# Score products of a windowed attention on quarters of the array, with queries stored plainly instead of as block-diagonal head pairs

## The chip, the cores and the metric

The kernel runs on one core of one Trainium2 chip. Times are device microseconds of one execution; the figure that counts is the median over several runs. A profiled execution gives the trace; its times count from the span's start.

## The reference, cut to what matters

Three layers follow one another: windowed attention, a layer of 8 experts of which each token uses 2, and a dense layer with 2048 hidden columns. The change touches the attention alone.

```python
# q, k, v: batch 4, 8 heads, 576 positions, 64 values a head
scores = scale * np.matmul(q, k.transpose(0, 1, 3, 2))
rel = pos[:, None] - pos[None, :]
mask = (rel >= 0) & (rel < 64)
scores = np.where(mask, scores, -1000000000.0)
scores = scores - np.max(scores, axis=-1, keepdims=True)
attn = np.exp(scores)
attn = attn / (np.sum(attn, axis=-1, keepdims=True) + 1e-09)
return np.matmul(attn, v)
```

## The kernel before

The 576 positions are 9 blocks of 64. A query of block i sees only keys of blocks i-1 and i, so a step s works on one block i = s // 4 of one batch b = s % 4 with all 8 heads: 36 steps. The 8 heads are 4 pairs (J = 4). Heads of a pair lie one above the other: the 64 values of the one on partitions 0 to 63, those of the other on 64 to 127. Queries and keys come transposed, so partitions are what a score product sums over.

A step's scores are one PSUM bank of 128 x 512: for pair j columns 128j to 128j+127 hold the 128 keys (two blocks of 64), and partitions hold 64 queries of the one head and 64 of the other. `scores(s)` (L917) first writes the mask there by a bf16 product with an identity (L932), then adds 4 fp32 products of full size (L936). For these to keep the heads apart, the stationary operand `q_bd` is block-diagonal: queries of the first head on partitions 0 to 63 and columns 0 to 63, of the second on partitions 64 to 127 and columns 64 to 127, and zeros elsewhere. VectorE writes the zeros once (L684, L685, four fills; the semaphore `zeroed`), and the loads fill in only the two diagonal parts.

TensorE's queue is written out by hand and works in order. In step s it does the scores of step s (L932, L936), transposes the probabilities of step s-2 (`transposed_probs`, L947), multiplies those of s-3 with the values (`values`, L959: 8 products of 64 stationary columns, going to output partitions 0 to 63 and 64 to 127 by turns), transposes the result of s-4 (`transposed_x`, L969), and in every second step forms the routing logits (`logits`, L978). VectorE takes the row maxima (L699), copies the transposed probabilities (L710) and scales the result (L723); ScalarE takes the exponentials (L552). Both also prepare the first expert's weights. Three banks hold scores, so the scores of step s wait for the exponentials of step s-3.

Queries come over SyncE's queue: block 0 in three parts by batch (0, 1, and 2 with 3), each as one transfer for either head (L289), then block 1 (`load_q`, L255, again two transfers a block), then keys. `q_bd` holds two blocks. ScalarE's queue loads the keys of blocks 0 and 1 in the same three parts (L569), and first values between them (L573). A part is complete when `row0_loaded` has counted its transfers. Before its first scores TensorE runs 12 filling products (L909).

Behind attention come routing on VectorE, gathers by GpSimd, then the expert and dense layers, whose products fill TensorE to the end.

Of the kernel before, what the change touches and what calls it, by code (L numbers as in the profile page):

```python
# [27 lines left out]
P = 128  # L28
# [17 lines left out]
def build(nc, qT, kT, vW, noise, w_gate, w_noise, w1, w2, w_in, w_out, out):  # L46
    BLOCKS, _, B, JQ = qT.shape
    Q = 64
    J = JQ // Q
# [6 lines left out]
    CH = 3  # L56
# [24 lines left out]
    with ExitStack() as ctx:  # L81
# [35 lines left out]

        with ExitStack() as s1:
            sb = sb_in(s1)
            q_bd = sb("q_bd", [P, 2, B, J, 2, Q])  # L120
            k_ring = sb("k_ring", [P, 4, B, JQ])
            v_ring = sb("v_ring", [P, B, D])
            probs = sb("probs", [P, CH, JQ * 2])
            probsT = sb("probsT", [P, J * P])
            xT_blk = sb("xT_blk", [P, 2, 2, 2, Q])
            negmax = sb("negmax", [P, 4, J])
            bias = sb("bias", [P, 4, J])
            rowsum = sb("rowsum", [P, 8, J])
            rowsum_g = sb("rowsum_g", [P, 2, J])
            rowinv = sb("rowinv", [P, 2, J])  # L130
            mask_first = sb("mask_first", [P, P], BF16)
            mask_odd = sb("mask_odd", [P, P], BF16)
            mask_even = sb("mask_even", [P, P], BF16)
            ident_b = sb("ident_b", [P, P], BF16)
            w_gn = sb("w_gn", [P, KD, 2 * E])
            x_blk = sb("x_blk", [P, CH, 2, JQ])
# [113 lines left out]
        @block.sync  # L250
        def _(sp):
            def load_q(r):
                for hi in range(2):
                    rows = slice(64 * hi, 64 * hi + 64)
                    sp.dma_start(q_bd[rows, r % 2, :, :, hi].rearrange("p b j q -> p (b j) q"),  # L255
                                 qT[r, rows].rearrange("p b (j q) -> p (b j) q", j=J)).then_inc(q_loaded[r % 2], 16)

            def load_k(r):
                sp.dma_start(k_ring[:, k_slot(r)], kT[r]).then_inc(k_loaded[r % 4], 16)

            def load_v(b, r):
                half = slice(64 * (r % 2), 64 * (r % 2) + 64)
                sp.dma_start(v_ring[half, b], vW[b, Q * r:Q * r + Q]).then_inc(v_loaded[b], 16)

            def store_x(t):
                for hi in range(2):
                    sp.dma_start(x_rows[P * t:P * t + P, JQ * hi:JQ * hi + JQ].rearrange("(u q) c -> q u c", u=2),
                                 x_blk[64 * hi:64 * hi + 64, t % CH]).then_inc(x_stored[t % CH], 16)

            def step(s):  # L270
                i, b = s // B, s % B

                if b == 1 and i + 2 < BLOCKS:
                    sp.wait_ge(scored, B * (i + 1))
                    load_q(i + 2)
                    if i >= 1 and i + 3 < BLOCKS:
                        load_k(i + 3)
                if i >= 1 and i + 1 < BLOCKS:
                    sp.wait_ge(pv_done, s + 1)
                    load_v(b, i + 1)  # L280
                if s % 2:
                    sp.wait_ge(x_ready, s + 1)
                    store_x(s // 2)


            for at in (slice(0, 1), slice(1, 2), slice(2, 4)):
                for hi in range(2):
                    rows = slice(64 * hi, 64 * hi + 64)
                    sp.dma_start(q_bd[rows, 0, at, :, hi].rearrange("p b j q -> p (b j) q"),  # L289
                                 qT[0, rows, at].rearrange("p b (j q) -> p (b j) q", j=J)  # L290
                                 ).then_inc(row0_loaded[at.start], 16)
            load_q(1)
            load_k(2)
            load_k(3)
            sp.dma_start(w_gn[:, :, 0:E], w_gate.rearrange("(a p) e -> p a e", p=P)).then_inc(gn_loaded, 16)
            sp.dma_start(w_gn[:, :, E:2 * E], w_noise.rearrange("(a p) e -> p a e", p=P)).then_inc(gn_loaded, 16)
            sp.dma_start(nz[:].rearrange("p t e -> p (t e)"), noise).then_inc(nz_loaded, 16)
            for s in range(G):
                step(s)


            sp.wait_ge(const_ready, ALL_CONSTANTS)
            for t in range(SURE, TILES):
                sp.dma_start(y_sorted[P * t:P * t + P], zeros[:]).then_inc(y_cleared, 16)

            def bounce(t, r, before):
                sp.wait_ge(gathered[r], before)
                sp.dma_start(x_sorted[bass.ds(P * t, P)], gath(r)).then_inc(bounced_r[r], 16)

            def confirm(r, count):  # L310
                sp.wait_ge(bounced_r[r], count)
                sp.sem_inc(bounced, 1)


            for t in range(DIRECT, DIRECT + LAG):
                bounce(t, t % GB, 16 * (t // GB) + 16)
            LOOPED = (TILES - DIRECT - LAG) // GB
            with sp.Fori(0, LOOPED) as m:
                for k in range(DIRECT, DIRECT + GB):
                    bounce(GB * m + k + LAG, (k + LAG) % GB, 16 * m + 16 * ((k + LAG) // GB) + 16)  # L320
                    confirm(k % GB, 16 * m + 16 * ((k - DIRECT) // GB) + 16)
            for t in range(DIRECT + GB * LOOPED, TILES):
                if t + LAG < TILES:
                    bounce(t + LAG, (t + LAG) % GB, 16 * ((t + LAG) // GB) + 16)
                confirm(t % GB, 16 * ((t - DIRECT) // GB) + 16)


            def keep(u, count):
                sp.wait_ge(y_stored[u], count)
                sp.sem_inc(y_kept, 1)  # L330

            sp.sem_inc(y_kept, 1)
            with sp.Fori(0, TILES // 2) as m:
                for u in range(2):
                    keep(u, 16 * m + 16)
            if TILES % 2:
                keep(0, 16 * (TILES // 2) + 16)


            with sp.Fori(0, GROUPS) as g:  # L340
                for u in range(TPG):
                    sp.wait_ge(o_copied, TPG * g + u + 1)
                    for h in range(2):
                        sp.dma_start(out[bass.ds(Q * g + S * (2 * u + h), Q)], o_out[Q * h:Q * h + Q, u]
                                     ).then_inc(o_stored[u], 16)
            for u in range(TPG):
                sp.wait_ge(o_stored[u], 32 * GROUPS)
# [332 lines left out]
        @block.vector  # L680
        def _(dve):

            for c in range(2):
                nc.vector.memset(q_bd[64:128, c, :, :, 0], 0.0).then_inc(zeroed, 1)  # L684
                nc.vector.memset(q_bd[0:64, c, :, :, 1], 0.0).then_inc(zeroed, 1)  # L685

            def low_piece(k):

                c, cols = k // PIECES, slice(PC * (k % PIECES), PC * (k % PIECES) + PC)
# [215 lines left out]
        def _(pe):  # L905
# [11 lines left out]
            def scores(s):  # L917
                i, b = s // B, s % B
                if i == 0:
                    pe.wait_ge(row0_loaded[min(b, 2)], 48)  # L920
                elif b == 0:
                    pe.wait_ge(q_loaded[i % 2], 32 * ((i + 1) // 2))
                    if i >= 2:
                        pe.wait_ge(k_loaded[i % 4], 16 * ((i + 2) // 4 if i % 4 >= 2 else i // 4))
                if s in (0, B):
                    pe.wait_ge(zeroed, 2 * i + 2)
                if s in (B, 2 * B):
                    pe.wait_ge(const_ready, ODD_CONSTANTS if i % 2 else EVEN_CONSTANTS)
                if s >= 3:
                    pe.wait_ge(exp_done, s - 2)  # L930
                mask = mask_first if i == 0 else mask_odd if i % 2 else mask_even
                nc.tensor.matmul(S_ps[s % CH][:].rearrange("p (j n) -> p j n", j=J), ident_b[:],  # L932
                                 mask[:].unsqueeze(1).to_broadcast([P, J, P]), start=True, stop=True)
                even, odd = (k_slot(max(i, 1) - (max(i, 1) + e) % 2) for e in range(2))
                for j in range(J):
                    mm = nc.tensor.matmul(  # L936
                        S_ps[s % CH][:, P * j:P * j + P], q_bd[:, i % 2, b, j].rearrange("p a q -> p (a q)"),
                        k_ring[:, even:odd + 1:odd - even, b, Q * j:Q * j + Q], start=False, stop=True,
                        skip_group_check=True)
                mm.then_inc(scored, 1)  # L940

            def transposed_probs(s):
# [53 lines left out]


            pe.wait_ge(const_ready, ALL_CONSTANTS)
            pe.wait_ge(zeroed, 5)
            keep_busy(banks[4], 28)  # L1000
            pe.wait_ge(route, ROUTE_PICKED)
            nc.tensor.matmul(R_ps[:, 0:(NT + 1) * E], upper[:], picked[:].rearrange("p t e -> p (t e)"), start=True,
# [174 lines left out]
```

## Time and profile before

| | |
|---|---|
| median of 3 runs | 1104.11 us (1103.42 to 1107.55) |
| the profiled execution | 1104.26 us, its span 1102.7 us |
| TensorE busy (matmul / weight load) | 98% / 85% of the span |
| VectorE, ScalarE, GpSimd busy | 32%, 31%, 32% |
| attention stage | from the start to about 122 us |
| last product of the routing logits | ends at 122.06 us |

TensorE is busy nearly all the time, so shares of busy time say little; what a stage is worth is read from the chain of work that ended last, which names at each moment what the end waited for. An fp32 product is recorded as two passes, each with a weight load (PEld) and a matmul (PE); an fp32 transpose as one. Matmul records overlap, since they are pipelined: their distance is the cost, not their length.

### The profile page before, as it was taken

How to read it: one execution, taken by the hardware profiler on the slowest of the kernel's cores; microseconds unless marked ns; L12 is line 12 of the kernel's file. 1: busy time of each engine (PE TensorE's matmuls, PEld its weight loads, DVE VectorE, ACT ScalarE, POOL GpSimd, SP SyncE). 2: the span in 40 equal slices, each digit the busy share in tenths (PEclk: the TensorE clock that was granted, in tenths of full speed). 3: DMA queues.
4: the chain of work that ended last, by engine and by line, in shares of the span. 5: the costliest groups of instructions: out<-in, count | busy, mean ns of one | idle time of the engine just before them, and what ended most of it. 6: DMA issues, size and time to landing. Idle time of an engine off the chain costs nothing.

```text
span 1102.7 us, 19553 instructions
## 1 busy us (share of the span) xinstructions
PE 1084.7 (98%) x6669; PEld 934.2 (85%) x6670; DVE 350.1 (32%) x685; ACT 345.3 (31%) x794; POOL 355.2 (32%) x230
## 2 busy tenths in 40 slices
PE   8999899999999999999999999999999999999998
PEld 6999568888888888888888887989989999899897
DVE  5888731122112211221122112424224132241321
ACT  4766212222222222222222221524325244252341
POOL 3000068559644628081725405921010110101000
PEclk8999989999999999999999999999999999999999
DMA  9886445995532514243333402220110201101000
GB/s 234 229 222 167 139 141 192 349 318 191 178 127 76 171 38 152 76 133 114 114 114 98 149 20 88 95 58 16 43 48 9 57 18 39 52 5 57 10 10 20
DMA packets 67844, 120.41 MB, mean 109 GB/s; under 512 B 25632, under 2 KB 30880, under 8 KB 67296
## 3 DMA queue, kind: packets, MB, share of 16 engines
q0 software_dynamic: 16688, 62.66, 17.4%
q1 hardware_dynamic: 37920, 33.67, 10.7%
q10 hardware_dynamic: 13200, 23.60, 6.6%
q8 instruction: 23, 0.38, 0.1%
q14 instruction: 13, 0.11, 0.0%
HBM read 87.14 MB, written 32.77 MB: 109 GB/s over the span
## 4 chain that ended last, share of the span: by engine, by line
PE 91%; POOL 4%; issue 3%; DMA 1%; DVE 0%; SPq 0%; ACT 0%; ACTq 0%; POOLq 0%; DVEq 0%
PE bank L1067 7%; PE bank L1065 7%; PE bank L1066 7%; PE bank L1050 7%; PE bank L1052 7%; PE bank L1051 7%; PE bank L1128 6%; PE bank L1130 6%; PE bank L1129 6%; PE bank L1115 6%; PE bank L1114 6%; PE bank L1113 6%; PE bank L1073 3%; PE bank L936 3%; PE bank L959 2%
## 5 line engine op out<-in xcount | busy, mean ns | idle before, releaser
L386 POOL TENSOR_TENSOR Wl<-stage,Wh 128x2048 fp32r<-128x2048 f32 x36 | 165.8, 4606 | 3.0
L1113 PE MATMUL bank<-zT_h,Wh 128*128 128x256 f32 x576 | 163.0, 283 | 1.0 <-DVE zT_l L873 1.0
L1115 PE MATMUL bank<-zT_h,Wl 128*128 128x256 f32 x576 | 163.0, 283 | 0.0
L1114 PE MATMUL bank<-zT_l,Wh 128*128 128x256 f32 x576 | 163.0, 283 | 0.0
L839 DVE COPY y_out<-bank 128x512 f32<-128x512 f32 x43 | 29.7, 692 | 359.7 <-PE bank L1067 342.4
L1050 PE MATMUL bank<-Wh,xT_h 128*128 x344 | 138.4, 402 | 1.1 <-POOL Wl L386 1.1
L1052 PE MATMUL bank<-Wh,xT_l 128*128 x344 | 134.6, 391 | 0.0
L1065 PE MATMUL bank<-Wh,hT_h 128*128 x344 | 133.9, 389 | 0.4 <-DVE hT_l L843 0.4
L1067 PE MATMUL bank<-Wh,hT_l 128*128 x344 | 134.2, 390 | 0.0
L1051 PE MATMUL bank<-Wl,xT_h 128*128 x344 | 133.8, 389 | 0.0
L1066 PE MATMUL bank<-Wl,hT_h 128*128 x344 | 133.8, 389 | 0.0
L620 ACT ACTIVATE hT_h<-bank 128x512 fp32r<-128x512 f32 x86 | 46.9, 596 | 260.9 <-PE bank L1073 153.4
L887 DVE SCALAR_TENSOR_TENSOR bank<-bank,square 128x512 f32<-128x512 f32 x72 | 50.4, 700 | 219.7 <-ACT square L659 219.7
L384 POOL CAST Wh<-stage 128x2048 fp32r<-128x2048 f32 x36 | 68.4, 1900 | 154.9 <-PE bank L1067 154.7
L502 POOL DMA_INDIRECT y_a<-y_sorted,pair_slot x18 | 17.2, 957 | 303.1 <-PE bank L1100 254.2
L1128 PE MATMUL bank<-Wh,gT_h 128*128 128x512 f32 x288 | 113.0, 393 | 0.2 <-POOL Wl L386 0.2
L1129 PE MATMUL bank<-Wl,gT_h 128*128 128x512 f32 x288 | 112.2, 390 | 0.0
L1130 PE MATMUL bank<-Wh,gT_l 128*128 128x512 f32 x288 | 112.2, 389 | 0.0
L1113 PEld LDWEIGHTS bank<-zT_h,Wh 128*128 128x128 f32 x576 | 110.5, 192 | 1.8 <-issue 1.5
L1114 PEld LDWEIGHTS bank<-zT_l,Wh 128*128 128x128 f32 x576 | 110.6, 192 | 0.3
L1115 PEld LDWEIGHTS bank<-zT_h,Wl 128*128 128x128 f32 x576 | 110.6, 192 | 0.0
L613 ACT ACTIVATE hid<-bank 128x512 f32<-128x512 f32 x86 | 51.4, 599 | 141.2 <-PE bank L1052 141.2
(154 smaller groups left out, 1674.0 us busy)
## 6 DMA issues: line engine op xcount, KB each, us to landing
stage<-w POOLq DMA_DIRECT2D x32, 1024.0 KB
y_sorted<-y_out ACTq DMA_DIRECT2D x43, 256.0 KB
x_in<-x_sorted ACTq DMA_DIRECT2D x39, 256.0 KB
x_sorted<-gath_b SPq DMA_DIRECT2D x20, 256.0 KB
x_sorted<-gath_a SPq DMA_DIRECT2D x19, 256.0 KB
x_rows<-x_blk SPq DMA_DIRECT2D x36, 128.0 KB, 3.0
out<-o_out SPq DMA_DIRECT2D x36, 128.0 KB, 2.2
q_bd<-qT SPq DMA_DIRECT2D x16, 256.0 KB, 4.3
```

Of the source, the lines that this page charges most:

```text
L1050: nc.tensor.matmul(H_ps[a][:], xT_h[:, u, k], high, start=(k == 0), stop=False)
L1051: nc.tensor.matmul(H_ps[a][:], xT_h[:, u, k], low, start=False, stop=False)
L1052: mm = nc.tensor.matmul(H_ps[a][:], xT_l[:, u, k], high, start=False, stop=(k == KD - 1))
L1065: nc.tensor.matmul(Y_ps[:], hT_h[:, k], high, start=(k == 0), stop=False)
L1066: nc.tensor.matmul(Y_ps[:], hT_h[:, k], low, start=False, stop=False)
L1067: mm = nc.tensor.matmul(Y_ps[:], hT_l[:, k], high, start=False, stop=(k == KF - 1))
L1113: nc.tensor.matmul(here, high, zT_h[:, k], start=(k == 0), stop=False)
L1114: nc.tensor.matmul(here, high, zT_l[:, k], start=False, stop=False)
L1115: mm = nc.tensor.matmul(here, low, zT_h[:, k], start=False, stop=(k == KD - 1))
L1128: nc.tensor.matmul(O_ps[u][:], gT_h[:, k, rows], Wh[:, 1, cols], start=(k == 0), stop=False)
L1129: nc.tensor.matmul(O_ps[u][:], gT_h[:, k, rows], Wl[:, 1, cols], start=False, stop=False)
L1130: mm = nc.tensor.matmul(O_ps[u][:], gT_l[:, k, rows], Wh[:, 1, cols], start=False, stop=(k == FC - 1))
```

## The change

Queries are stored plainly in `q_ring` (128 partitions, two blocks), in one transfer a part instead of two. For each pair of heads there are two products in place of one, each with 64 rows, 64 stationary columns (queries) and 128 moving columns (keys): head 0 on the array's rows 0 to 63 and columns 0 to 63, head 1 on rows 64 to 127 and columns 64 to 127. The output's place is the same. The four fills and the waits for them go; semaphore counts follow.

```diff
-            q_bd = sb("q_bd", [P, 2, B, J, 2, Q])
+            q_ring = sb("q_ring", [P, 2, B, JQ])
...
             def load_q(r):
-                for hi in range(2):
-                    rows = slice(64 * hi, 64 * hi + 64)
-                    sp.dma_start(q_bd[rows, r % 2, :, :, hi].rearrange("p b j q -> p (b j) q"),
-                                 qT[r, rows].rearrange("p b (j q) -> p (b j) q", j=J)).then_inc(q_loaded[r % 2], 16)
+                sp.dma_start(q_ring[:, r % 2], qT[r]).then_inc(q_loaded[r % 2], 16)
...
             for at in (slice(0, 1), slice(1, 2), slice(2, 4)):
-                for hi in range(2):
-                    rows = slice(64 * hi, 64 * hi + 64)
-                    sp.dma_start(q_bd[rows, 0, at, :, hi].rearrange("p b j q -> p (b j) q"),
-                                 qT[0, rows, at].rearrange("p b (j q) -> p (b j) q", j=J)
-                                 ).then_inc(row0_loaded[at.start], 16)
+                sp.dma_start(q_ring[:, 0, at], qT[0, :, at]).then_inc(row0_loaded[at.start], 16)
...
-            for c in range(2):
-                nc.vector.memset(q_bd[64:128, c, :, :, 0], 0.0).then_inc(zeroed, 1)
-                nc.vector.memset(q_bd[0:64, c, :, :, 1], 0.0).then_inc(zeroed, 1)
...
             def scores(s):
                 i, b = s // B, s % B
                 if i == 0:
-                    pe.wait_ge(row0_loaded[min(b, 2)], 48)
+                    pe.wait_ge(row0_loaded[min(b, 2)], 32)
                 elif b == 0:
-                    pe.wait_ge(q_loaded[i % 2], 32 * ((i + 1) // 2))
+                    pe.wait_ge(q_loaded[i % 2], 16 * ((i + 1) // 2))
...
-                if s in (0, B):
-                    pe.wait_ge(zeroed, 2 * i + 2)
...
                 for j in range(J):
-                    mm = nc.tensor.matmul(
-                        S_ps[s % CH][:, P * j:P * j + P], q_bd[:, i % 2, b, j].rearrange("p a q -> p (a q)"),
-                        k_ring[:, even:odd + 1:odd - even, b, Q * j:Q * j + Q], start=False, stop=True,
-                        skip_group_check=True)
+                    for hi in range(2):
+                        rows, head = slice(Q * hi, Q * hi + Q), slice(Q * j, Q * j + Q)
+                        mm = nc.tensor.matmul(S_ps[s % CH][rows, P * j:P * j + P], q_ring[rows, i % 2, b, head],
+                                              k_ring[rows, even:odd + 1:odd - even, b, head], start=False, stop=True,
+                                              skip_group_check=True)
                 mm.then_inc(scored, 1)
...
-            pe.wait_ge(zeroed, 5)
+            pe.wait_ge(zeroed, 1)
```

TensorE's queue in block 1, before (a row names line, output and inputs, and the output's partitions and columns of one product):

```order
L932 MATMUL bank<-mask_odd,ident_b 128x512
L936 MATMUL bank<-k_ring,q_bd 128x128 x4
L947 MATMUL bank<-ident,probs 128x128 x4
L959 MATMUL bank<-v_ring,probsT 64x64 x8
L969 MATMUL bank<-ident,x_blk 128x2x64 x2
L978 MATMUL bank<-w_gn,xT_blk 128x16 x4
```

The same place after:

```order
L919 MATMUL bank<-mask_odd,ident_b 128x512
L925 MATMUL bank<-k_ring,q_ring 64x128 x8
L935 MATMUL bank<-ident,probs 128x128 x4
L947 MATMUL bank<-v_ring,probsT 64x64 x8
L957 MATMUL bank<-ident,x_blk 128x2x64 x2
L966 MATMUL bank<-w_gn,xT_blk 128x16 x4
```

Nothing changes its place; the four score products are eight with half the output partitions each, between the mask and the transposes, which both use the whole array.

SyncE's queue at the start, before (rows give the shape of a transfer's target):

```order
L289 DMA q_bd<-qT 64x4x64 x4
L289 DMA q_bd<-qT 64x8x64 x2
L255 DMA q_bd<-qT 64x16x64 x2
L259 DMA k_ring<-kT 128x1024 x2
L295 DMA w_gn<-w_gate 128x4x8
L296 DMA w_gn<-w_noise 128x4x8
```

And after:

```order
L284 DMA q_ring<-qT 128x256 x2
L284 DMA q_ring<-qT 128x512
L253 DMA q_ring<-qT 128x1024
L256 DMA k_ring<-kT 128x1024 x2
L288 DMA w_gn<-w_gate 128x4x8
L289 DMA w_gn<-w_noise 128x4x8
```

Eight query transfers in rows of 64 values are four in whole rows, so the key loads stand four transfers nearer to the front.

## Rows read from the trace of the kernel before

**Rows 1.** The page: span.

```profile
span 1102.7 us, 19553 instructions
```

**Rows 2.** The page: chain that ended last, by line.

```profile
PE bank L1067 7%; PE bank L1065 7%; PE bank L1066 7%; PE bank L1050 7%; PE bank L1052 7%; PE bank L1051 7%; PE bank L1128 6%; PE bank L1130 6%; PE bank L1129 6%; PE bank L1115 6%; PE bank L1114 6%; PE bank L1113 6%; PE bank L1073 3%; PE bank L936 3%; PE bank L959 2%
```

**Rows 3.** Chain in order of time, 59.8 to 66 us: start, length, what.

```profile
59.99 0.21 PE bank L932
60.20 0.89 PE bank L936 x8
61.09 0.44 PE bank L947 x4
61.53 0.62 PE bank L959 x16
62.14 0.37 PE bank L969 x2
62.51 0.80 PE bank L978 x8
...
65.85 0.21 PE bank L932
```

**Rows 4.** Stretch, its length, busy PE, PEld, DVE, ACT, POOL.

```profile
60.00:112.00 52.00, 52.00 (x622) 47.25 (x623) 43.44 (x116) 35.66 (x160) 1.46 (x2) 1.00 0.69 188
```

**Rows 5.** Timeline of TensorE within one step's value products.

```profile
61.68 0.46 PE L959 MATMUL bank<-v_ring,probsT 128*64 128x64 f32 x10
...
61.86 0.29 PE L959 MATMUL bank<-v_ring,probsT 128*64 128x64 f32 x4
```

**Rows 6.** Who waited for whom, 0 to 130 us: total, times, longest.

```profile
PEld bank L959 <- issue: 5.9, 35, 0.2
```

**Rows 7.** Timeline, 0 to 22 us.

```profile
1.23 4.17 PE L909 MATMUL bank<-ones_b 128*128 128x512 bf16 x12 [1.23 <-POOL ones_b L410]
...
2.57 0.62 ACTq L569 DMA_DIRECT2D k_ring<-kT x1
...
4.80 0.91 DVE L685 MEMSET q_bd<- 64x1024 f32 x1 [0.27 <-issue]
...
8.06 0.59 PE L932 MATMUL bank<-mask_first,ident_b 128*128 128x512 bf16 x1 [2.66 <-POOL upper L434]
...
10.96 0.61 PE L932 MATMUL bank<-mask_first,ident_b 128*128 128x512 bf16 x1 [0.61 <-DMA q_bd<-qT]
...
13.94 0.61 PE L932 MATMUL bank<-mask_first,ident_b 128*128 128x512 bf16 x1 [0.67 <-DMA q_bd<-qT]
```

**Rows 8.** Chain in order of time, 0 to 24 us.

```profile
4.46 9.43 DMA q_bd<-qT
...
13.94 0.61 PE bank L932
14.55 1.71 PE bank L936 x8
```

**Rows 9.** DMA issues of 0 to 17 us: count, size, median us to landing.

```profile
k_ring<-kT ACTq DMA_DIRECT2D x2, 256.0 KB, 4.3
k_ring<-kT ACTq DMA_DIRECT2D x1, 512.0 KB, 7.2
...
q_bd<-qT SPq DMA_DIRECT2D x4, 64.0 KB, 6.1
```

**Rows 10.** DMA queues (q1 SyncE, q10 ScalarE), 3 to 14 us: packets, MB, share.

```profile
q10 hardware_dynamic: 1223, 1.93, 60.3%
q1 hardware_dynamic: 3532, 0.88, 47.9%
```

**Rows 11.** GB/s of all queues in 40 slices of 0 to 17 us.

```profile
GB/s 0 0 0 0 0 166 233 254 215 255 195 80 228 228 277 277 315 387 348 334 270 335 317 284 299 289 268 230 217 203 170 168 188 221 234 202 207 223 318 357
```

**Rows 12.** Stretches as in rows 4; behind POOL the granted clock.

```profile
7.60:17.70 10.10, 8.36 (x34) 7.39 (x35) 3.09 (x7) 3.48 (x19) 3.29 (x11) 0.50 1.18 271
17.80:38.00 20.20, 20.20 (x242) 18.16 (x241) 16.82 (x46) 14.40 (x68) 0.81 (x2) 1.00 0.98 243
```

## The prediction

> **What bounds the kernel now.** I read the page first: the span is 1102.7 us [rows 1]; the chain that ended last is TensorE nearly everywhere, and the line that the change rewrites, L936, holds 3% of it [rows 2]. The run of this profile took 1104.26 us, 0.15 us above the median of the three timed ones, so I add to 1104.26. I then took the attention stage alone, by the chain in order of time. A step there is a sum of TensorE pieces and nothing else: mask 0.21, scores 0.89 (8 passes of 0.111 us: each of the 4 products is recorded twice), transposed probabilities 0.44, values 0.62, transposed x 0.37, and every second step 0.80 for the logits [rows 3]. Two steps make 2 x 2.53 + 0.80 = 5.86 us, and the trace's period (a mask piece at 59.99, the next of the same kind at 65.85) is 5.86 us. So TensorE alone sets the pace. In 52 us of this stage VectorE is busy 43.4 us and ScalarE 35.7 us [rows 4]: a longer TensorE step is not hidden by them, and a shorter one could gain at most 0.49 us of 2.93 before VectorE takes over. The steps from the fifth on, 32 of 36, run in this regime; the first four are different.
>
> **The score products.** Before: 4 products a step, full array, 128 columns moving, two passes each, 0.111 us a pass. After: 8 products a step on diagonal quarters, still 128 columns moving, so 16 passes. The moving length decides: the transposes too take 0.11 us for 128 columns [rows 3]. If the two quarters of a pair run together, 8 pairs x 0.111 = 0.89 us, exactly as before; the halved weight load buys nothing. That two tiles can run together is seen in the value products, which go to alternate column halves: from the record at 61.68 with 10 passes left to that at 61.86 with 4 left, 3 pairs pass in 0.18 us, 0.06 us a pair [rows 5], and 64 columns at the rate of 0.111 us for 128 are 0.056 us. Were they serial it would be 0.11 us a pair. For quarters that differ in rows as well no row exists. Bounds: 0.47 us a step (16 passes at the 0.03 us that half a value pair costs) and 1.78 us (16 x 0.111). I take 0.89, because the value products are the nearest row and share with the new ones what matters: different output partitions, one bank.
>
> **Changing the tiling.** Value products are the only ones now that don't use the whole array. On entering them the weight load stands idle 0.17 us, 35 times out of 36 [rows 6]: nothing is loaded ahead. In the chain the piece of 8 pairs takes 0.62 us, of which 8 x 0.06 = 0.48 is work, so entering costs 0.14 us. The two x transposes behind them take 0.37 us where two of the four probability transposes take 0.22: leaving costs 0.15 us. The change puts two more such borders in each step, mask to scores and scores to transposes: 0.29 us, taken as 0.30 since the idle load says 0.17. Nothing covers it, since TensorE never waits here. Bounds: 0 (a row split needs no emptying, or the mask product hides it) and 0.40. 32 steps x 0.30 = 9.6 us, and 0.3 us for the fourth step; in the first three TensorE waits for data anyway. Together +9.9 us.
>
> **Query loads.** Before, each block of queries is two transfers in pieces of 256 bytes (64 values); after, one transfer of 128 rows of 4 KB, the same bytes. In steady state it is hidden: no wait of TensorE on q_bd after the start. SyncE saves one issue a block, which nobody waits for. At the start it matters. The first step's mask starts at 8.06, the second's at 10.96, the third's at 13.94, the last two released by the q_bd transfer [rows 7]. For the first the view names a constant of GpSimd that scores don't wait for; q_bd's 64 KB transfers, landing 6.1 us after their issue [rows 9], fit. The chain has 9.43 us from the last issue to its landing [rows 8]. The keys on ScalarE's queue, of 256 KB, land after 4.3 us while q_bd's 64 KB need 6.1 [rows 9]. Between 3 and 14 us SyncE's queue moves 0.88 MB in 3532 packets, ScalarE's 1.93 MB in 1223 [rows 10]: many small packets take turns with few large ones. After, the queries of row 0 are 384 packets of 1 and 2 KB instead of 2048. Then the first step is held by the filling products, which end at 5.40 [rows 7]: 2.7 us earlier. The second can follow at about 7.5. The third needs the last keys (512 KB on ScalarE's queue, issued at 2.57 [rows 7], landing 7.2 us later: 9.8 [rows 9]). But these now take turns with packets of 4 KB, since block 1's queries and the next key blocks are issued early. ScalarE's queue must move 1.3 MB up to its last keys; if packets go in turn, SyncE's moves row 0's queries (0.5 MB), block 1's (0.5) and a key block (0.5) in that time: 2.9 MB. Data flows from 2.1 us on, the sixth slice of 0.425 us, and the slices go up to 387 GB/s [rows 11]. At the mean of 255 GB/s (2.81 MB in 11 us, [rows 10]) the last keys are in at 13.5 us, at 350 GB/s at 10.4. I take 320 GB/s, nearer to the good slices since the small packets are gone: 11.2 to 11.3 us against 13.94, 2.6 us gained. Bounds: 0 (the third step still starts at 13.94) and 5 us (third step at 9.8, and the clock). The clock: it is at 0.50 from 7.6 to 17.7 and full behind that [rows 12], after TensorE had idled from 5.40 to 8.06. At half clock mask and scores of the third step take 0.61 + 1.71 = 2.32 us [rows 8] against 1.10 at full [rows 3]. Less idling may bring the clock back earlier by a step, 1.2 us; that is in the upper bound, not in the sum.
>
> **The zeroing.** Four VectorE fills of 0.91 us go, the last ended at 5.71, before the first scores [rows 7]: nothing now. They were ready before the data, and after the change they would have stood at 5.71 against 5.40, so leaving them out is what allows the 5.40, 0.3 us of the gain above. The wait for zeros behind the stage stays with a count that its own fill meets.
>
> **The sum.** 1104.26 + 9.9 - 2.6 = 1111.6; I say 1111.5. Bounds of this case: borders 0.25 to 0.35 us each pair (8.2 to 11.5), start 0 to 5: 1107.5 to 1116. Behind attention everything is a chain through the last scores (routing, gather, first expert), so the shift goes through in full.
>
> **The rivals.**
> A. Pairs run together, borders are paid: the forecast, 0.66.
> B. The quarters of a pair don't run together. They read different rows but write one bank: 16 x 0.111 = 1.78 us of scores a step, +0.89 x 33 = 29.4 us on top, less the same start: 1141. For it: no row shows two row groups at once. Against: value pairs share a bank and overlap [rows 5]. 0.14. The Trainium skill, TensorEngine Tiling (Array Packing), Restrictions and Gotchas, says that different row tiles cannot access the same PSUM bank at once; by that rule this rival comes true, because both quarters of a pair go to one bank. No row of this kernel uses row tiles, so the trace can't confirm it; I hold the rule to be about tiles above one another, and this is my doubt, not a measurement.
> C. The new borders cost nothing (mask and scores flow into each other): only the start counts, 1099 to 1104, forecast 1101.7. For it: nothing; against it both borders of the values. 0.10.
> D. Faster: narrower quarters also shorten the passes, to 0.47 us a step. Then a step gains 0.42 and pays 0.30: -0.12 x 33 = -4.0, with the start -6.6: 1097.7. It decides once the scores' piece is under 0.59 us. Against it: the pass goes by moving columns, which stay 128. 0.05.
> E. The lower clock: if half-used arrays made the clock fall to 0.50 in this stage, TensorE's 2.93 us steps would double: +90 us and more. Value products, too, use part of the array a time, and the clock stands at 1.00 throughout [rows 12]. 0.03, and 0.02 for the unforeseen.
>
> **The numbers.** About 0.5% (5.5 us) is what a measurement of this kernel can tell from no change: 1098.6 to 1109.6. Of A some four fifths lie above 1109.6, since it takes borders and start both at their good end to come below. Slower: 0.53 + 0.14 + 0.03 + 0.01 = 0.71. Same: 0.13 + 0.10 = 0.23. Faster: D and a very good start, 0.06. The range leaves out B, E and the rest (0.19) and holds A, C and most of D: 1096 to 1118, A's own being 1107.5 to 1116.
>
> **What would show it.** In the chain of the changed kernel: a scores piece of 16 passes at 1.04 us (0.89 and the entry) and the transposes behind it at 0.59 in place of 0.44; a period of 6.46 us for two steps; an idle weight load ahead of the scores, some 0.17 us in every step; first mask at 5.4, third at 11.3; the stage's end (last logits) 7 us later than 122. A period near 8.2 us is B, one of 5.86 is C. The forecast is wrong if passes are bound by something other than moving columns, or if the start gains over 4 us.

## The result, and the profile after

The changed kernel takes 1113.86 us (median of 7 runs, 1111.96 to 1115.61) against 1104.12 us (7 runs): the ratio is 1.0073, 95% interval [1.0058, 1.0089]. It is slower by 9.7 us by the medians and by 8.1 us by the means, which is what the ratio says; the forecast was 7.4 us, and the range held the time. The two figures differ because the runs of the kernel before fall into a lower and an upper group (1103.4 to 1104.1 us and 1107.6 to 1108.6 us here), and the median lies in the lower one. Beside this comparison and those of the experiments the kernel before was run 94 times, with a median of 1105.5 us; against that the changed kernel is 8.4 us slower. The profiled execution is the slowest of the seven, 1115.61 us with a span of 1114.0 us, so its trace shows some 2 us more than the median.

The chain in order of time, changed kernel, one step with logits and the mask of the next (start, length, what), answers to [rows 3]:

```profile
62.12 0.21 PE bank L919
62.34 1.02 PE bank L925 x16
63.36 0.59 PE bank L935 x4
63.94 0.62 PE bank L947 x16
64.56 0.37 PE bank L957 x2
64.93 0.80 PE bank L966 x8
65.73 0.22 PE bank L919
```

Only two pieces differ from before: the scores took 0.89 us and take 1.02, the transposes behind them took 0.44 and take 0.59. This is what the prediction named (1.04 and 0.59). The step is 0.28 us longer; two steps take 6.42 us, where 6.46 was forecast. There are 16 records now instead of 8, but they come in pairs: in this step two start 0.007 us apart (at 62.425 and 62.432 us), and one pair follows the other after 0.109 us. So eight pairs take the 0.89 us that eight full-size passes took, and 0.13 us is the entry.

Where the 0.28 us lie is seen in the waits for nothing but issue, changed kernel, 0 to 135 us:

```profile
PEld bank L925 <- issue: 10.3, 36, 0.4
PEld bank L935 <- issue: 6.5, 33, 0.8
...
PEld bank L947 <- issue: 5.9, 35, 0.2
```

Before, such a wait stood in every step at the value products alone [rows 6]. Now the weight loads of the scores (L925) and of the transposes behind them (L935) have it too, once a step. In the records of one step the first weight load of each of these groups starts only with its first product (62.264 and 62.265 us for the scores, 63.284 and 63.287 for the transposes, 63.871 and 63.873 for the values), while inside the transposes the load runs 0.11 us ahead of its product. So no weights are loaded ahead across a change of the array's form: whole array, 64x64 quarters, or halves of the columns as in the value products. The idle time of the load is not the price. It is 0.29 us ahead of the scores on the mean (0.17 was forecast), but the piece in the chain is only 0.13 us longer.

The start, TensorE's timeline of the changed kernel, answers to [rows 7]:

```profile
5.71 0.38 PE L919 MATMUL bank<-mask_first,ident_b 128*128 128x512 bf16 x1
...
7.04 0.39 PE L919 MATMUL bank<-mask_first,ident_b 128*128 128x512 bf16 x1
...
11.86 0.61 PE L919 MATMUL bank<-mask_first,ident_b 128*128 128x512 bf16 x1 [3.40 <-DMA k_ring<-kT]
```

The first three masks start at 5.71, 7.04 and 11.86 instead of 8.06, 10.96 and 13.94. The third is no longer held by queries but by the last keys. The fifth starts at 17.79 us, where it was 19.58: the start gains 1.8 us in this pair of traces. One pair of traces is a rough measure of it: among the traces of kernels whose start is not changed, the fifth mask comes anywhere from 17.5 us (e7 below) to 20.0 (e8).

From the fifth mask to the 36th 99.2 us pass instead of 90.5: 8.7 us for 31 steps. From the last mask to the first product of the last logits it is 10.9 us in both. With 1.8 us gained, these logits start 6.8 us later than before (127.82 against 121.00). So two fifths of the 11.3 us by which the span is longer lie behind attention. The routing stage shows more than half of that, TensorE's timeline, first before:

```profile
121.91 6.20 PE L909 MATMUL bank<-ones_b 128*128 128x512 bf16 x28
128.79 0.24 PE L1002 MATMUL bank<-picked,upper 128*128 128x152 bf16 x1 [0.68 <-DVE picked L770]
```

and in the changed kernel:

```profile
127.82 1.81 PE L966 MATMUL bank<-w_gn,xT_blk 128*128 128x16 f32 x8 [0.69 <-ACT xT_blk L554]
129.47 8.80 PE L898 MATMUL bank<-ones_b 128*128 128x512 bf16 x28
138.11 0.23 PE L990 MATMUL bank<-picked,upper 128*128 128x152 bf16 x1
```

and its clock in two stretches (stretch, length, busy times, granted clock, DMA share, GB/s):

```profile
128.00:134.70 6.70, 6.70 (x21) 3.39 (x22) 3.74 (x13) 2.03 (x3) 0.00 (x0) 0.50 0.86 311
...
148.50:158.60 10.10, 10.10 (x45) 5.48 (x43) 5.74 (x30) 0.00 (x0) 3.28 (x4) 0.50 0.18 52
```

TensorE was granted half its clock (1.2 of 2.4 GHz) from 127.9 to 134.8 us, behind the last waits of attention. The 28 filling products (L898), which are there to keep it busy while VectorE works out the routing, then take 8.80 us, where they took 6.20 in the trace of before, and the first product that matters (L990) has no wait before it: it comes when the filling ends, 1.8 us after VectorE's last result for it (136.31 us). The last logits themselves take 1.81 us instead of 1.06. Together the ranks, which L990 begins, stand 10.3 us behind the last logits' start instead of 7.8. Whether this fall of the clock belongs to the change is a question for e3 to e7. Another 2.0 us of the 11.3 come later: at half clock TensorE spends 10.2 us there instead of 6.8, and its waits behind 150 us add up to 4.4 us instead of 3.4, with one of 1.4 us for which the profile names nothing.

### The profile page after: what moved, and what is told of

It reads as the page before. It is cut to its first block, busy times and chain, and to the rows that moved or that the text cites. A ratio compares the mean times of both kernels' runs of the same rounds, so it can differ in the third digit from the quotient of the medians.

```text
span 1114.0 us, 20113 instructions
## 1 busy us (share of the span) xinstructions
PE 1096.4 (98%) x6957; PEld 928.8 (83%) x6958; DVE 347.5 (31%) x681; ACT 345.5 (31%) x794; POOL 355.6 (32%) x230
## 4 chain that ended last, share of the span: by engine, by line
PE 94%; POOL 3%; DVE 1%; issue 1%; DMA 1%; ACT 0%; ACTq 0%; DVEq 0%; POOLq 0%
PE bank L1038 7%; PE bank L1040 7%; PE bank L1053 7%; PE bank L1055 7%; PE bank L1039 7%; PE bank L1054 7%; PE bank L1116 6%; PE bank L1117 6%; PE bank L1118 6%; PE bank L1103 6%; PE bank L1102 6%; PE bank L1101 6%; PE bank L1061 3%; PE bank L925 3%; PE bank L947 2%; PE bank L935 2%
```

## The experiments

The border theory: each change of the array's form (whole, quarters, column halves) costs TensorE about 0.14 us, whatever the products; passes cost by their moving columns, and two quarters run together. Rivals are in the expectations. Every time below is a median; every ratio is to the kernel before, whose runs were taken beside the experiment, so it need not be the quotient of two medians.

**Quarters alone (e1).** The change's products on the old storage.

```diff
-                    mm = nc.tensor.matmul(
-                        S_ps[s % CH][:, P * j:P * j + P], q_bd[:, i % 2, b, j].rearrange("p a q -> p (a q)"),
-                        k_ring[:, even:odd + 1:odd - even, b, Q * j:Q * j + Q], ...)
+                    for hi in range(2):
...
+                        mm = nc.tensor.matmul(S_ps[s % CH][rows, P * j:P * j + P], q_bd[rows, i % 2, b, j, hi],
+                                              k_ring[rows, even:odd + 1:odd - even, b, head], ...)
```

> The score products on quarters, with the block-diagonal storage, its fills and its loads kept. Border theory: two more crossings between the whole array and a tiled form in each of 36 steps, 0.28 to 0.30 us a step where TensorE never waits (33 steps): about 9.3 us over the kernel before, and nothing gained at the start (third mask still at 13.9 us). With the routing stage's reaction to the clock 9 to 13 us. Rival, that the loads cost the time: within 2 us of the kernel before.

Measured: 1115.38 us, ratio 1.0095 [1.0076, 1.0115]. The fifth to the 36th mask take 99.2 us, as in the changed kernel. The products alone carry the whole loss. The changed kernel, with the plain storage on top, is 1.5 us faster than this one (give or take 1.1).

**Storage alone (e4).**

```diff
-                    for hi in range(2):
...
-                        mm = nc.tensor.matmul(S_ps[s % CH][rows, P * j:P * j + P], q_ring[rows, i % 2, b, head], ...)
+                    pair = slice(P * (j // 2), P * (j // 2) + P)
+                    mm = nc.tensor.matmul(S_ps[s % CH][:, P * j:P * j + P], q_ring[:, i % 2, b, pair], ...)
```

> Plain storage and its four loads, no fills, but four full-size score products a step that read 128 neighbouring query columns. The scores then mix the two heads of a pair, so values and routing differ from the reference; number and shape of all instructions are those of the kernel before. Border theory: no borders added, only the earlier start: third mask at 11.9 us against 13.9, so 1.7 to 3 us under the kernel before (1101 to 1102.5). Rival, that plain loads themselves slow the stage: above 1104.

Measured: 1101.73 us, ratio 0.9969 [0.9950, 0.9987], 90.5 us from the fifth to the 36th mask, the third mask at 12.04. The two parts of the change have opposite signs: by the ratios +0.95% (e1) and -0.31% (e4). Their sum of 0.64% is near the 0.73% of the whole change; each of the three is uncertain by some 0.2%. This kernel leaves out the separation of the heads, so its routing, and with it the work of the expert stage, can differ: only its attention stage can be set against the others, and there it starts the last logits 2.6 us before the kernel before.

**Two more borders without any quarter (e3).** Full-size scores; only the value products are split around the transposes.

```diff
+                if 3 <= s < G + 3:
+                    values(s - 3, 0)
                 if 2 <= s < G + 2:
                     transposed_probs(s - 2)
                 if 3 <= s < G + 3:
-                    values(s - 3)
+                    values(s - 3, 1)
```

> The kernel before, with the eight value products of a step issued as four ahead of the transposes and four behind them: two more crossings a step and no other change (same products, same shapes, full-size scores). Border theory: +0.29 us a step, 9 to 10.5 us over the kernel before, in all 1113 to 1117. Rival, that the quarters of the scores themselves (row split) are what costs: no change, 1104.

Measured: 1114.42 us, ratio 1.0090 [1.0071, 1.0108]. The chain of this kernel (L960 are the value products, L947 the transposes of the probabilities):

```profile
61.53 0.89 PE bank L936 x8
62.42 0.38 PE bank L960 x8
62.80 0.59 PE bank L947 x4
63.38 0.38 PE bank L960 x8
63.77 0.37 PE bank L971 x2
64.13 0.22 PE bank L932
```

Two halves of 0.38 us instead of one piece of 0.62, and the transposes at 0.59 instead of 0.44: 0.29 us a step, with the same products in the same shapes. That shows the price to be the border's, not the quarters'. The last logits start 9.9 us later than in the kernel before, and the span is 9.6 us longer: here, with full clock at that place, the shift goes through as it is.

**Borders between two tiled forms (e5).** The changed kernel, values moved ahead of the transposes.

```diff
-                if 2 <= s < G + 2:
-                    transposed_probs(s - 2)
                 if 3 <= s < G + 3:
                     values(s - 3)
+                if 2 <= s < G + 2:
+                    transposed_probs(s - 2)
```

> The changed kernel with the value products of a step moved ahead of the transposes, right behind the quarter scores: three changes of form a step (whole to quarters, quarters to column halves, column halves to whole) instead of four. If every change of form costs the same 0.14 us: 0.14 x 33 = 4.7 us less than the changed kernel, about 1109. Rival, that only leaving or entering the whole array costs: two borders less, 9 us less, about 1104.5. Rival, that the changed form costs by row split alone: no change.

Measured: 1108.37 us, ratio 1.0024 [1.0001, 1.0047], 5.5 us under the changed kernel by medians. From the fifth to the 36th mask 94.6 us pass instead of 99.2: 0.15 us a step for one border less. Its chain:

```profile
61.45 0.22 PE bank L919
61.67 1.02 PE bank L925 x16
62.69 0.61 PE bank L947 x16
63.31 0.59 PE bank L935 x4
63.90 0.22 PE bank L957 x2
```

The x transposes fall from 0.37 to 0.22 us, but the values right behind the quarter scores still take 0.61 us, 0.14 of it the entry. Going from quarters to column halves costs as much as leaving the whole array; neither rival holds. Here too the clock is full behind the last logits, and the ranks stand 7.8 us behind their start.

**Do the quarters run together (e2).** The four products of one head first, then the other's.

```diff
-                for j in range(J):
-                    for hi in range(2):
+                for hi in range(2):
+                    for j in range(J):
```

> The changed kernel with the four products of the first head issued before the four of the second, so neighbours in the queue share a quarter. If the 0.89 us of the scores rest on two quarters running together because they stand side by side in the queue, the scores' piece becomes 16 x 0.111 = 1.78 us plus 0.13: +0.78 to 0.89 us a step, 28 to 32 us over the changed kernel (about 1143). Rival, that the passes would be short anyway or are reordered: unchanged, 1113.9.

Measured: 1132.58 us, ratio 1.0241 [1.0215, 1.0267], 18.7 us over the changed kernel. The chain and the clock at the start:

```profile
61.05 0.22 PE bank L919
61.27 1.51 PE bank L925 x16
62.78 0.59 PE bank L935 x4
```

```profile
12.30:29.20 16.90, 16.90 (x109) 13.33 (x108) 6.01 (x15) 5.08 (x26) 0.93 (x1) 0.50 0.41 131
```

Neighbours on one quarter don't run together: the piece grows by 0.49 us. But not to the 1.91 I expected: with 0.13 for the entry 1.38 are left, 12.4 passes of 0.111 us. The records show how: the first head's start at 61.20, 61.36 and then every 0.109 us to 62.02, and the second head's first starts at 61.69 already, when three of the first head's eight have yet to start. The row of the clock adds something not asked for: in this stretch TensorE is busy all the time, and is granted half its clock, from 12.2 to 29.3 us, in the changed kernel only from 11.9 to 15.3. So the fifth mask comes 3.2 us later than in the changed kernel, and the steps up to 29 us are longer for the clock too, not for the order alone.

**Less filling in the routing stage (e6, e7).** The same cut in the changed kernel (e6) and in the one before (e7).

```diff
-            keep_busy(banks[4], 28)
+            keep_busy(banks[4], 14)
...
-            keep_busy(banks[4], 28)
+            keep_busy(banks[4], 14)
...
-            keep_busy(banks[4], 16)
+            keep_busy(banks[4], 8)
```

> The changed kernel with the filling products of the routing stage cut from 28, 28 and 16 to 14, 14 and 8. In the changed kernel's trace the clock is at half there and 28 products take 8.8 us instead of 6.2, so that the ranks wait for filling: if that is the cause of the 2 to 4 us beyond attention, this one ends 2 to 4 us earlier than the changed kernel (1110 to 1112). Rival: with less filling the clock falls more often and the first expert's products run at half clock: no gain or 2 us worse.

> The same cut of the filling products in the kernel before. There the ranks don't wait for filling in its trace; the runs of the kernel before lie at 1103.3 to 1104.3 and at 1107.3 to 1110. If the upper ones come from filling at half clock, the upper group disappears and the median is 1102 to 1104. Rival, the clock falls more often: 1105 to 1108.

Measured: e6 1111.28 us (9 runs, 1109.45 to 1114.48), 2.6 us under the changed kernel; e7 1103.47 us (12 runs, 1101.67 to 1105.98), ratio 0.9984 [0.9968, 1.0000]. In e6 the clock is at half at the same place, but the ranks now wait for VectorE:

```profile
129.15 5.96 PE L898 MATMUL bank<-ones_b 128*128 128x512 bf16 x14
136.04 0.24 PE L990 MATMUL bank<-picked,upper 128*128 128x152 bf16 x1 [0.93 <-DVE picked L759]
```

The ranks come 8.4 us behind the last logits' start instead of 10.3. So filling at half clock does cost 1.9 us in the trace of the changed kernel. But the kernel before gains as much from the cut: by means e6 is 2.1 us under the changed kernel (give or take 1.4) and e7 is 1.9 us under the kernel before (give or take 1.2). With the cut in both, the change costs 7.9 us (give or take 1.2; 0.76% by the two ratios), without it 8.1 us (0.73%). So filling at half clock is no measurable part of what the change costs. The traces fit this: the fall of the clock doesn't go with the change. e7 has the clock at half from 119.5 to 126.3 us; the kernel before, e3 and e4 have it full behind their last logits; of the kernels with quarters e1 and e6 have it at half, as the changed one has, and e5 has it full. That the upper runs vanish in e7 (1105.98 at most, where the kernel before went to 1110.79) is what was expected. That those were runs with filling at half clock is likely but not shown, since no trace of one was kept.

**Fewer borders than before (e8 to e10, e15, e16).** If borders are the price, the kernel before, which pays two in every step, can save some. e8 keeps full-size scores and issues the values of two steps together; it needs a second buffer for the transposed probabilities, and the x transposes, logits and casts come one step later.

```diff
+                if s % 2:
+                    for k in (s - 4, s - 3):
+                        if 0 <= k < G:
+                            values(k)
                 if 2 <= s < G + 2:
                     transposed_probs(s - 2)
-                if 3 <= s < G + 3:
-                    values(s - 3)
-                if 4 <= s < G + 4:
-                    transposed_x(s - 4)
+                if 5 <= s < G + 5:
+                    transposed_x(s - 5)
```

> The kernel before with full-size scores, but the value products of two steps issued together in every second step (two buffers for the transposed probabilities; x transposes, logits and the first expert's casts one step later): one pair of borders in two steps instead of two. Border theory: 0.29 us less for 17 of the pairs, 4.9 us under the kernel before. Rival: VectorE, 84% busy in the stage and now uneven between steps, becomes late and takes the gain: 0 to 2 us.

Measured: 1107.82 us, ratio 1.0028 [1.0012, 1.0044]: slower than before. The border's part came as expected in steady state; the chain of e8 shows 32 passes of values in one piece:

```profile
62.69 0.89 PE bank L940 x8
63.59 1.08 PE bank L963 x32
64.67 0.59 PE bank L951 x4
65.25 0.22 PE bank L973 x2
```

1.08 us for two steps' values instead of 1.24, and two x transposes at 0.22. Two steps take 5.56 us, 0.30 less. But from the fifth to the 36th mask only 1.7 us are gained, not 4.5, and 1.6 of them only because the last of these steps has no values in it: they follow behind the last mask, from where 12.0 us instead of 10.9 pass to the last logits' start. So nearly the whole saving is lost inside the stage, in a few steps. Two gaps ahead of the values (0.85 us at 56.0, 0.86 at 57.6) end just as the last parts of two value loads land (56.77 and 58.33 us); VectorE's copies were done before 55.8. The mask at 101.4 us waits 1.1 us for a load of queries. SyncE issues value loads when the values before have been used, and between them stores x when it is ready; with values in pairs both come later. The trace of the kernel before has no such wait. Then comes the stage's end, into a clock at half from 120.3 to 127.1 us and 28 fillings: the ranks stand 10.0 us behind the last logits' start instead of 7.8. What the pairs saved per step went to loads that came too late and to a longer way out.

e9 adds block 0 on quarters, e10 the short filling.

```diff
                 for j in range(J):
+                    if i == 0:
+                        for hi in range(2):
+                            mm = nc.tensor.matmul(S_ps[s % CH][rows, P * j:P * j + P], q_first[rows, b, head], ...)
+                        continue
```

> As e8, and block 0 alone (the four first steps, in three of which TensorE waits for data anyway) stored plainly and scored on quarters, the rest full-size. Border theory with the start's measured gain of 1.8 us, less one step's border: 1.5 us under e8. Rival: two more VectorE fills of 0.46 us in the fifth step delay the chain: no gain over e8.

> As e9, with the filling products of the routing stage cut from 28, 28 and 16 to 14, 14 and 8 as in e7. By what e7 gave, about 2 us under e9 and about 8.5 us under the kernel before (ratio 0.992). Rival: the clock's fall comes at another place and costs what it saves: as e9.

Measured: e9 1104.83 us, ratio 1.0000 [0.9982, 1.0018], 3.0 us under e8. One of its twelve runs took 3398 us and is left out of the ratio; why is open, since the trace is of another run. e10: 1101.11 us, ratio 0.9967 [0.9955, 0.9980], faster than both kernels, but by about half of the 8.5 us expected. In e9 and e10 too TensorE waits twice for a load of queries inside the stage (2.4 and 1.7 us in all).

Two variants tell what in e10 is worth its price: e15 is e10 without the pairs, e16 is e10 with the last steps one by one again (the end of the loop over steps, not shown).

> The kernel before, with block 0 alone stored plainly and scored on quarters and the filling cut to 14, 14 and 8; value products as before, every step. From e9's trace the start gains more than 1.8 us when no step is held (the fifth mask at 14.0 us in place of 19.6), and e7 gave 2 us: 5 to 8 us under the kernel before, 1097.5 to 1100. If pairing in e10 was worth its price, this one is 2 us or more behind e10; if pairing lost in the tail what it saved, level with e10 or ahead.

> As e10, but in the last steps (from step 36 on) values, x transposes and logits follow one by one again, so that the pairing doesn't lengthen the stage's end. In the traces of e8 and e10 the last logits come 13.5 us after the last mask, in the kernel before 11.7: 1.8 us under e10, about 1099. Rival: ScalarE's copies in the tail hold it anyway, as e10.

Measured: e15 1103.23 us, ratio 0.9975 [0.9961, 0.9989]; e16 1101.78 us, ratio 0.9960 [0.9939, 0.9982]. e15 fell short by more than 3 us. Its start, TensorE's timeline (L935 the mask), is as hoped:

```profile
7.75 0.39 PE L935 MATMUL bank<-mask_first,ident_b 128*128 128x512 bf16 x1
...
9.30 0.39 PE L935 MATMUL bank<-mask_first,ident_b 128*128 128x512 bf16 x1
```

The third mask starts at 9.30, the fifth at 13.95, 5.6 us earlier than before. But the waits of the same kernel show who gives it back:

```profile
ACT Wh L542 <- DMA stage<-w: 4.2, 1, 4.2
```

ScalarE casts the first expert's weights between the exponentials and is now there before the weights are; the exponentials queue behind the cast, and from the fifth to the 36th mask 94.1 us pass instead of 90.5. In e7, where the fifth mask came at 17.5 us, the same wait is 1.7 us; the kernel before has none. So beside single values block 0 on quarters brings nothing measurable: e15 is 0.5 us under e7, give or take 1.0. On top of the pairs (e9 against e8) it was 2.9 us by means, give or take 2.3. The pairs are worth 2.0 us once the filling is short (e10 against e15, give or take 1.1). e16 doesn't differ measurably from e10, and its profiled run, its slowest, can't show why.

## Why the prediction was right

**The score products.** Right: 8 pairs in 0.89 us, exactly the full-size products' time. e2 shows that this rests on two quarters running together. Rival B is out, and so is D: a pair of passes with halved rows and columns takes 0.109 us, as a full-size pass does. The rule of the Trainium skill that the prediction put beside B (TensorEngine Tiling (Array Packing), Restrictions and Gotchas: different row tiles can't access one PSUM bank at once) does not hold as written in this trace: both quarters of a pair use one bank, and the trace has them start 0.007 us apart. They write different partitions; tiles above one another were not tried.

**The borders.** Right, and the heart of the case: 0.28 us a step measured, 0.30 forecast, 8.7 us over 31 steps where the sum had 9.9 for 33; behind the last mask nothing was added. e1, e3 and e5 make it a price of the change of form alone. The value products, read in the trace of before, had given both its halves.

**The query loads.** The direction was right, the size too large: 1.8 us gained by the fifth mask in the traces, 1.5 us by the runs (the changed kernel against e1), against 2.6 forecast. The third mask came at 11.86 where 11.3 was forecast, held by the keys:

```profile
k_ring<-kT ACTq DMA_DIRECT2D x1, 512.0 KB, 9.3
...
q_ring<-qT SPq DMA_DIRECT2D x2, 128.0 KB, 3.4
```

In this view of the changed kernel's transfers the last keys take 9.3 us instead of 7.2 [rows 9], the first queries 3.4 instead of 6.1, as the turn-taking with large packets had it. The experiments agree: with block 1's queries in whole rows the last keys land after 9.3 and 9.4 us (changed kernel, e4), with block 0 plain and block 1's queries still in small pieces after 6.5 to 6.7 (e9, e10, e15, e16), and there the third mask starts at 9.1 to 9.3.

**The sum.** At the last logits the traces stand 6.8 us apart, where the sum had 7.3. Part of this closeness is luck: the borders were put 1.2 us too high and the start 0.8 us too high, with opposite signs. Behind attention "the shift goes through in full" holds where the clock stays full: in e3, e4 and e5 the ranks stand 7.8 us behind the last logits' start, as before. It does not hold between the two traces the case began with, where filling at half clock and slower logits add 2.5 us. The prediction did not look at the filling. But e6 and e7 show that cutting the filling gives both kernels the same, and by means the change costs 8.1 us (6.4 to 9.8), 0.7 more than forecast. The 9.7 us of the medians owes the rest to a median of the kernel before that fell among its lower runs. The 2.0 us that the profiled run of the changed kernel loses further back, with half clock for longer and one wait of 1.4 us, stay open in their cause; e3's trace has no such loss.

The zeroing was not tried apart; in the trace of before its fills ended at 5.71 us, ahead of the first scores, as said. Rivals C and E are out: the borders are paid, and the clock stood at full for all of the steady stage, from 15.3 to 127.9 us.

## What to carry to other kernels

Count the changes of the array's form in a step, not the share of the array that is used: here a smaller product that moves as many columns took as long, and two more changes of form cost 0.28 us in a step of 2.9. Put products of one form together, but look at which loads are issued later by the regrouping, and at the stage's end, where a longer pipeline is paid once but in full. A gain at the start is worth only what the next thing in line, here a weight transfer ahead of the exponentials on ScalarE, lets through; and products that only fill must be so few that they don't hold the real ones even at half clock. And before a difference between two traces is put down to a change, see whether a run of the old kernel can have it too: the same edit on both kernels (e6, e7) told that here.

## What the runs showed that I had not expected

TensorE starts products of another quarter three passes ahead of their order in its queue (e2: 1.38 us instead of 1.78 behind the entry). In that kernel the granted clock stayed at 0.50 for 17 us at the start, with TensorE busy without a gap; in no other trace is it more than 10.2 us there. Whether it is the single quarter at work that holds it was not tried apart. And with plain queries for block 0 alone, TensorE kept its full clock through the start (e9: full from 5.3 to 97.5 us), while in the kernel before it fell at 7.5:

```profile
6.00:97.00 91.00, 85.59 (x1063) 79.06 (x1063) 74.00 (x196) 61.50 (x283) 7.17 (x19) 1.00 0.90 236
```

Its fifth mask comes at 14.0 us, 5.5 us earlier than before, where 1.8 were expected. Against the changed kernel (11.86 and 17.79 us) the third mask is 2.6 us earlier, where the earlier keys show, and the two steps behind it are 1.1 us shorter, at full clock where the changed kernel has half until 15.3 us. Much of this didn't reach the end: from the fifth to the 36th mask e9 takes 91.8 us where e8 takes 88.8, with a wait of 1.9 us for the weights and the waits for queries.
